# Attention stage: the row maxima are subtracted by a TensorE product, the exponential reads PSUM, and the four engines' orders change

## What is computed

```python
batch, n_heads, seq, head_dim = (4, 8, 576, 64)          # factor = 4, Sd = 144
q_d, k_d, v_d = means over 4 neighbouring rows of q, k, v
out_up = np.repeat(sm_attn(q_d, k_d, v_d), factor, axis=2)
mask = np.abs(pos[:, None] - pos[None, :]) < factor      # a band 7 wide
scores = np.where(mask, scale * q @ k.T, -1e9)
scores = scores - np.max(scores, axis=-1, keepdims=True)
attn = np.exp(scores)
attn = attn / (np.sum(attn, axis=-1, keepdims=True) + 1e-09)
out = (out_up + attn @ v).astype(np.float32)
x = out as (2304, 512)
for w_in, w_out, g in ((512x2048, 2048x512, 1.0), (the same shapes, 1.702)):
    h = x @ w_in;  x = (h / (1 + exp(-g * h))) @ w_out
```

## Time and profile before

| | us |
|---|---|
| median of 3 runs (808.9 to 809.27) | 809.27 |
| the profiled execution | 808.21 |
| its span in the profile | 806.4 |
| attention, up to the first feed-forward product at 100.55 | about 101 |
| busy over the span: PE / DVE / ACT / POOL | 790.0 / 646.0 / 530.8 / 208.8 |

### The profile page before, as it was taken

How to read it: one execution, slowest core, us unless ns; L and a number is a source line. 1 busy time by engine, 2 the same in 40 slices (tenths; PEclk the granted TensorE clock), 3 DMA queues, 4 the chain that set the end, 5 groups by cost and what they waited for, 6 DMA issues and landing times.

```text
span 806.4 us, 15771 instructions
## 1 busy us (share of the span) xinstructions
PE 790.0 (98%) x5864; PEld 763.4 (95%) x5864; DVE 646.0 (80%) x905; ACT 530.8 (66%) x849; POOL 208.8 (26%) x203
## 2 busy tenths in 40 slices
PE   9888799999999999999999999999999999999998
PEld 5666599999999999999999999999999999999998
DVE  7999899999898778998678898899555688456466
ACT  5878865677655678555687556678455786465673
POOL 5899977520274220445200000000000000000000
PEclk9999999999999999999999999999999999999999
DMA  8877647787878887677877778868887877878773
GB/s 282 266 249 238 197 150 259 262 298 233 283 236 268 260 315 245 217 261 258 289 267 249 239 250 262 256 224 272 306 275 257 273 249 266 304 250 271 264 256 136
DMA packets 100763, 205.51 MB, mean 255 GB/s; under 512 B 8784, under 2 KB 56400, under 8 KB 100688
## 3 DMA queue, kind: packets, MB, share of 16 engines
q1 hardware_dynamic: 100688, 204.51, 76.0%
HBM read 160.96 MB, written 43.52 MB: 254 GB/s over the span
## 4 chain that ended last, share of the span: by engine, by line
PE 88%; POOL 8%; issue 3%; DVE 1%; ACT 0%; POOLq 0%; DVEq 0%
PE hid L351 43%; PE yp L377 42%; POOL vpair L1038 2%; POOL vavg L1042 1%; PE yp L393 1%; POOL pband L1032 1%; POOL G L1062 1%; POOL G L1063 1%; POOL G L1068 1%; POOL G L1066 1%; POOL x L284 0%; DVE wh L315 0%; PE sc L1342 0%; PE hp L1342 0%; PE pt L1229 0%
## 5 line engine op out<-in xcount | busy, mean ns | idle before, releaser
L351 PE MATMUL hid<-xs,wh 128*128 128x384 f32 x2016 | 351.3, 334 | 0.7 <-issue 0.4
L351 PEld LDWEIGHTS hid<-xs,wh 128*128 128x128 f32 x2016 | 349.3, 188 | 1.7 <-issue 1.4
L377 PE MATMUL yp<-gr,wh 128*128 128x384 f32 x1968 | 342.1, 334 | 0.0
L377 PEld LDWEIGHTS yp<-gr,wh 128*128 128x128 f32 x1968 | 341.2, 188 | 0.1
L306 ACT ACTIVATE wh<-wr 128x1024 fp32r<-128x1024 f32 (+1 forms) x164 | 164.6, 1004 | 149.8 <-PE hid L351 120.0
L569 DVE TENSOR_TENSOR gr<-G,gr 128x768 fp32r<-128x768 f32 x144 | 137.9, 964 | 52.7 <-ACT gr L449 52.7
L449 ACT ACTIVATE gr<-G 128x768 fp32r<-128x768 f32 x144 | 121.8, 845 | 66.9 <-PE yp L377 66.8
L315 DVE TENSOR_TENSOR wh<-wr,wh 128x1024 fp32r<-128x1024 f32 x76 | 95.1, 1251 | 19.0 <-ACT wh L306 18.8
L412 ACT ACTIVATE G<-G 128x1152 f32<-128x1152 f32 x48 | 55.7, 1161 | 0.8 <-DVE G L564 0.8
L533 DVE TENSOR_TENSOR hv<-p,hid 128x384 f32<-128x384 f32 x48 | 26.3, 548 | 29.8 <-PE hid L351 28.0
L559 DVE TENSOR_TENSOR G<-hv,hid 128x384 f32<-128x384 f32 x48 | 26.3, 549 | 28.2 <-PE hid L351 28.2
(11 more groups left out here) (101 smaller groups left out, 748.0 us busy)
## 6 DMA issues: line engine op xcount, KB each, us to landing
wh<-rests SPq DMA_DIRECT2D x72, 512.0 KB, 3.7
wr<-sums_out SPq DMA_DIRECT2D x48, 512.0 KB, 4.7
wr<-in_w_out SPq DMA_DIRECT2D x36, 512.0 KB, 5.2
rests<-wh SPq DMA_DIRECT2D x36, 512.0 KB, 3.5
wr<-sums_in SPq DMA_DIRECT2D x40, 384.0 KB, 4.0
wr<-in_w_in SPq DMA_DIRECT2D x40, 256.0 KB, 3.5
qk<-in_qkT SPq DMA_DIRECT2D x11, 576.0 KB, 4.8
G<-in_w_in SPq DMA_DIRECT2D x12, 512.0 KB, 5.3
```

Source lines behind the costliest of these rows:

```text
L351: last = eng.matmul(hid[:, at, 0:HALF], lhsT=wh[:, w % SLOTS, part, a % 4, cc * P:(cc + 1) * P], rhs=xs[:, rest, q, cc, :], start=start an ...
L377: last = eng.matmul(yp[:, at + m, 0:HALF], lhsT=wh[:, w % SLOTS, part, p % 4, m * P:(m + 1) * P], rhs=gr[:, p, rest, :], start=start and p ...
```

## The change

The constant `less`, the negated identity, is built in f32 in a spare part of the tile `yt`. VectorE's subtraction is gone. In its place TensorE adds two f32 products to the PSUM tile `sc`: `less` times the maxima, each maximum broadcast over its 64 columns (`band_less`). ScalarE's exponential reads `scores` in PSUM instead of `pband` and writes `pband` as before. So `sc` is free for the next unit only after the exponential (`b_exp`), no longer after the subtraction.

The orders change with it. TensorE runs both score steps first, then all four transposed groups, then `band_less`, then the products with v. ScalarE makes all four copies ahead of the exponential, and `normalise` ahead of `early`. VectorE runs `sums` for the next unit ahead of the sums of the exponentials, except in the units of `RESTS` and `RESTS_W` (4, 6, 8, 10, 12, 14), where it stays behind the reciprocal.

```diff
+            less = spare[:, HALF * P:HALF * P + P]
...
+            eng.memset(less, 0.0).then_inc(consts_fill, 1)
...
+            identity(less, -1.0)
...
             def body(u, first, last):
                 old = u.before()
                 if not first:
-                    for j in range(NLG):
+                    for j in range(NG):
                         group(old, j)
                 if last is not None:
                     eng.wait_ge(b_sub, u.n + 1)
-                    eng.activation(probs[u.odd], probs[u.odd], ACT.Exp, scale=scale_band).then_inc(b_exp, 1)
+                    eng.activation(probs[u.odd], scores.rearrange("p (b n) -> p b n", n=P), ACT.Exp,
+                                   scale=scale_band).then_inc(b_exp, 1)
...
-                if not first:
-                    for j in range(NLG, NG):
-                        group(old, j)
...
+                if last is not None and u.n:
+                    normalise(u)
                 if not first:
                     early(u.n)
-                if last is not None and u.n:
-                    normalise(u)
...
-                    eng.wait_ge(b_max, u.n + 1)
-                    eng.tensor_tensor(e, scores.rearrange("p (b s n) -> p b s n", s=2, n=WIN),
-                                      mxb[:].rearrange("p (b s) -> p b s", s=2).unsqueeze(3).broadcast_to(e.shape),
-                                      ALU.subtract).then_inc(b_sub, 1)
...
+                busy = u.n in RESTS or u.n in RESTS_W
                 if not first:
                     early(u.n)
                 if last is not None:
+                    if not last and not busy:
+                        sums(u.after())
                     eng.wait_ge(b_exp, u.n + 1)
...
-                    if not last:
+                    if not last and busy:
                         sums(u.after())
...
-                eng.wait_ge(b_sub, u.n)
+                eng.wait_ge(b_exp, u.n)
...
+            def band_less(u):
+
+                eng.wait_ge(b_max, u.n + 1)
+                for a in (0, HALF):
+                    last = eng.matmul(scores[:, a * WIN:(a + HALF) * WIN], lhsT=less,
+                                      rhs=mxb[:, a:a + HALF].unsqueeze(2).broadcast_to([P, HALF, WIN]),
+                                      start=False, stop=True, skip_group_check=True)
+                last.then_inc(b_sub, 1)
...
                 else:
                     band_scores(u)
+                    avg_scores(u)
                 if u.n == 1:
                     keep_warm(IDLE[1], pt)
-                if not first:
-                    for j in range(NLG):
+                if first:
+                    eng.wait_ge(consts, 4)
+                else:
+                    for j in range(NG):
                         group(old, j)
                 if last is not None:
-                    avg_scores(u)
+                    band_less(u)
                 if first:
                     keep_warm(IDLE[0], pt)
-                    eng.wait_ge(consts, 3)
-                if not first:
-                    for j in range(NLG, NG):
-                        group(old, j)
+                else:
                     band_product(old)
                     avg_product(old)
```

More of the change, by code:

```diff
@@ L890, in build @@
             sma = sb("sma", [AR, NA, 2])
-            spare = ffn.spare(HALF * P + SD)
-            ptb, oavg = spare[:, 0:HALF * P].rearrange("p (t n) -> p t n", t=HALF), spare[:, HALF * P:]
+            spare = ffn.spare(HALF * P + P + SD)
+            ptb, oavg = spare[:, 0:HALF * P].rearrange("p (t n) -> p t n", t=HALF), spare[:, HALF * P + P:]
+            less = spare[:, HALF * P:HALF * P + P]
             pta = sb("pta", [P, 2, NA * AR])
@@ L1001, in _, with identity @@
         def _(eng):
-            def identity(tile):
-                eng.affine_select(out=tile[:], in_=tile[:], compare_op=ALU.not_equal, fill=1.0, base=0,
+            def identity(tile, value=1.0):
+                eng.affine_select(out=tile, in_=tile, compare_op=ALU.not_equal, fill=value, base=0,
                                   pattern=[[-1, P]], channel_multiplier=1).then_inc(consts, 1)
@@ L1009, in _ @@
             eng.memset(ident[:], 0.0).then_inc(consts_fill, 1)
-            eng.wait_ge(consts_fill, 3)
-            fills = 3
+            eng.memset(less, 0.0).then_inc(consts_fill, 1)
+            eng.wait_ge(consts_fill, 4)
+            fills = 4
             for sign in (1, -1):
@@ L1020, in _ @@
             eng.sem_inc(consts, 1)
-            identity(ident16)
+            identity(ident16[:])
             eng.wait_ge(consts, 2)
-            identity(ident)
+            identity(less, -1.0)
             eng.wait_ge(consts, 3)
+            identity(ident[:])
+            eng.wait_ge(consts, 4)
             def body(u, first, last):
@@ L1161, in body @@
                 if last is not None:
-                    e = probs[u.odd].rearrange("p b (s n) -> p b s n", n=WIN)
                     eng.wait_ge(band_sc, 2 * (u.n + 1))
@@ L1316, in body @@
                 if last is None:
-                    eng.wait_ge(b_sub, UNITS)
+                    eng.wait_ge(b_exp, UNITS)
                     eng.wait_ge(a_exp, NA * UNITS)
```

## The result

The changed kernel takes **821.22 us** (median; 821.16 to 821.26), the kernel before 809.09 in the same comparison: a ratio of 1.0152, 95% interval 1.0135 to 1.0170. Slower by 12.1 us, where the forecast was 821.3.

What follows compares the result with a forecast made beforehand. TensorE is busy 98% of the span; in the attention VectorE, then GpSimd, is full. Start +3.0, 14 units +10.1 (86.1 + 3.2 + 4.75 against 83.9) and end -1.1 make +12.0: 821.3 us, range 812.5 to 825.5.

Steps and rivals of the forecast that it cites:

- What bounds the kernel: Feed-forward part: TensorE is never idle there, so what the attention gains or loses arrives in the total one for one.
- The price of the pair: TensorE's two new f32 products of 320 columns: 1.08 us, or 1.20 from start to the next group's start.
- bf16 price: Rival, chance 0.07: the pair on TensorE costs 0.28 us, loop 5.35, about -1 us with waits, middle 806.9.
- TensorE's loop: One attention unit on TensorE, start to start: 6.15 us against 5.99 before; fourteen loops are 86.1 us.
- `sums` behind the reciprocal: Six units of `RESTS` and `RESTS_W`: TensorE's scores over means wait 0.5 us for VectorE's sums, 3.2 rounded in all.
- Rounding behind `normalise`: ScalarE's `early` delays the copy freeing the transposes' bank: 0.3 us in units 3, 5, 9, 11, 13, 0.5 in 7.
- Where both waits meet: Units 10, 12 and 14: `normalise` waits behind `sums`, then the copy comes late, costing 1.0, 1.0 and 0.75 us.
- The start: Units 0 and 1: the exponential of unit 1 comes at 16.56 instead of 13.53, +3.0 us.
- The end: After unit 15's exponential, those over means follow by 1.95 us instead of 3.06, -1.1 us.
- One sign: Changed profile: GpSimd was to be seen waiting for `rcb` in every unit.
- The exponential from PSUM: ScalarE's exponential reading PSUM was taken as equal: cost 0, between -0.1 and +0.1 us a unit.
- Only the loop counts: Rival, chance 0.15: ScalarE's and VectorE's waits vanish in slack, leaving +4.1 us, 813.4.

Runs made afterwards that it cites:

- sums ahead everywhere: The changed kernel with VectorE's sums for the next unit ahead of the sums of the exponentials in every unit: 816.44 us, ratio 1.0094.
- f32, both waits gone: The changed kernel, f32 product kept, with VectorE's sums ahead in every unit and ScalarE's rounding ahead of normalise: 814.60 us, ratio 1.0071.
- rounding before normalise: The changed kernel with ScalarE's feed-forward rounding ahead of normalise again, as before the change: 817.69 us, ratio 1.0107.
- GpSimd relieved alone: The kernel before, with the differences of x of units 7 to 14 made by VectorE instead of GpSimd: 809.15 us, ratio 1.0004.

## Why the prediction was right, point by point

- **What bounds the kernel.** The attention's delay arrived in full: 12.0 us at the first feed-forward product, 12.1 in the medians.
- **The price of the pair**, 1.08 us, against the bf16 price of 0.28: the profile has 1.19 from start to start (forecast 1.20), and the doubled product cost 1.08 per unit. The bf16 pair came to about 0.26. The Trainium skill's page FP8 and Floating Point Precision (TensorE Precision Notes) has true FP32 at four passes; the price bears this out, four times that of the bf16 pair, though the trace shows two records per product and not four. The product formula of the Trainium skill's page VectorE: DVE Perf Modes (the TRN2 errata section), 6 cycles plus one per column, is right for the bf16 pair here and a quarter of the f32 one.
- **TensorE's loop**, 6.15 us: 6.20 measured in the units without entries.
- **`sums` behind the reciprocal**, 0.53 per unit: units 4, 6 and 8 took 6.73. Right.
- **Rounding behind `normalise`**, 0.3 in five units, 0.5 in unit 7: 6.42 and 6.63 measured, so 0.2 and 0.4. Where both waits meet I had 1.0, 1.0 and 0.75 on top of 0.53 and the measured intervals of units 10, 12 and 14 are 7.17, 7.38 and 7.17, so 0.44, 0.65 and 0.44 on top. This term was oversized: 4.75 forecast, 3.0 measured, and 3.0 is also what the run with the rounding first gave back. The 14 units together: 9.1 instead of 10.1, as each loop is 0.05 longer than forecast.
- **The start**, +3.0: +3.86. From the maximum of unit 0 to the exponential of unit 1 it is +3.13, nearly the forecast. The other 0.73 is how much later that maximum starts in this execution (6.86 before, 7.59 after), because TensorE's products ahead of it ran slowly for longer (last section); the forecast took the clock as the same. **The end**, -1.1: -0.97.
- So the total was met to 0.1 us by luck: misses of 0.9 and 1.0 cancel, and 0.73 of the first is the state of one execution. Without it the change costs 11.3 us in the attention by these two profiles, where the medians differ by 12.1; the profiles do not place the remaining 0.8. Each term was right in kind and sign.
- **One sign did not come**: GpSimd was to wait for `rcb` in every unit; it did so 10 times in 14, and from unit 8 on only in every other one.
- **The exponential from PSUM** at no cost: 0.71 us instead of 0.74, a gain of 0.03.
- **The rivals.** "Only the loop counts" (813.4) is near what the f32 kernel takes with both waits gone, 814.6. The bf16 price was forecast at 806.9 as the middle, and measured at 808.43 with the waits, 808.25 without: no verdict either way against the kernel before, where the rival had mostly "faster".

## What to carry to other kernels

Work moved from a full engine to one with 0.8 us to spare must cost less than those 0.8 us, in the type in which it is moved: here a subtraction of 0.83 us became a pair of products of 1.08 us in f32 and of 0.26 in bf16, and the values allowed bf16. Add the receiving engine's start-to-start distances over one iteration before you look at the other one's relief. When two engines are nearly full, as VectorE and GpSimd were, freeing one may show nothing until it takes work from the other; here it did not.

## What the runs showed of the hardware that I had not expected

The filler products at the start of the program, 512 columns each, come 0.43 us apart at first, 1.2 columns per ns; the same products later come 0.22 us apart, 2.4 columns per ns (seven in 1.68 - 0.17 us). I read these as the two levels of TensorE's clock, 1.2 and 2.4 GHz, though the clock column reads 1.00 in both stretches. Before, the last two of the first kind stand at 4.80 and 5.09, the second sooner than 0.43 behind the first:

```profile
4.80 0.45 PE L1342 MATMUL hp<-zeros 128*128 128x512 bf16 x1
5.09 0.38 PE L1342 MATMUL sc<-zeros 128*128 128x512 bf16 x1
```

After, the spacing of 0.43 lasts up to the mask products of unit 0:

```profile
5.23 0.63 PE L1351 MATMUL sc<-zeros 128*128 128x512 bf16 x1
5.66 0.74 PE L1235 MATMUL sc<-band,ident 128*128 128x320 bf16 x2
```

The local scores behind them are late by as much, and so is their maximum, which stands at 6.86 before:

```profile
7.59 0.82 DVE L1166 TENSOR_REDUCE mxb<-sc 128x10 f32<-128x640 f32 x1 [1.55 <-PE sc L1244]
```

It goes by execution and not by kernel. The exponential of unit 0 starts at 9.91, 9.84 and 9.94 in the profiles of the changed kernel and of two others with the f32 product ("sums ahead everywhere" and "f32, both waits gone"), and at 8.73 in a third whose unit 0 is the same ("rounding before normalise"). In "GpSimd relieved alone", whose unit 0 is that of the kernel before, the maximum starts at 7.58 and not at 6.86. From that maximum to the exponential of unit 1 both f32 kernels, early and late, take 9.80 us. So up to 1.2 us of the spread between executions can come from here.

Of the 1.0 us more in the feed-forward layers, 0.61 is one wait: TensorE stood that long ahead of 207.99 in the profile after, for VectorE's rest of the gates (L569), and not at all at that place in the profile before. Which of VectorE's and ScalarE's instructions come first there was not tested.

```profile
207.99 1.28 PE L377 MATMUL yp<-gr,wh 128*128 128x384 f32 x6 [0.61 <-DVE gr L569]
```

The pause of 1.74 us in the middle of a group of products stays unexplained, and so does that of 0.82 us in "f32, both waits gone": no semaphore releases them in the trace.
